# A threshold search without its second product, moved into the first layers of each expert, with w1 in three buffers and the last expert written out

## What is computed

```python
logits = x @ w_gate                      # 3072 x 8
order = np.argsort(-logits.flatten())
for idx in order:                        # greedy: best score first
    tok, e = idx // E, idx % E
    if assigned[tok] >= 0 or counts[e] >= cap: continue
    assigned[tok] = e; counts[e] += 1    # cap = 3072 // 8 = 384
for e in range(E):
    h = np.maximum(x[mask_e] @ w1[e], 0.0)   # w1: 384 x 1024
    out[mask_e] = h @ w2[e]                  # w2: 1024 x 384
y = ((x @ w_a) * (x @ w_b)) @ w_out          # 384 x 1536, 1536 x 384
```

## Time and profile before

| | us |
|---|---|
| median of 3 runs | 1288.75 |
| the profiled execution | 1286.86 |
| its span | 1285.1 |
| PE busy | 1134.4 (88%) |
| DVE busy | 880.1 (68%) |
| POOL busy | 615.1 (48%) |
| ACT busy | 519.2 (40%) |
| attention | about 0 to 420 |
| round 0 alone | about 421 to 483 |
| eight experts | about 483 to 1270 |
| last scatters | 1270.8 to the end |

### The profile page before, as it was taken

The page is one execution under the profiler, slowest core; times in us unless marked ns, Lnnn a source line. Parts: engine busy times, 40 slices in busy tenths (PEclk is TensorE's granted clock), DMA queues, the critical chain, the costliest instruction groups (busy, mean ns, idle before and its releaser), DMA issues.

```text
span 1285.1 us, 38287 instructions
## 1 busy us (share of the span) xinstructions
PE 1134.4 (88%) x14896; PEld 1017.9 (79%) x14896; DVE 880.1 (68%) x1789; ACT 519.2 (40%) x968; POOL 615.1 (48%) x598
## 2 busy tenths in 40 slices
PE   2899999999998319999999999989989999999995
PEld 1577777777777218898988988989889889898894
DVE  6889999999997664765565566565565565575573
ACT  6767777777773213223214214214213213213212
POOL 5667677776664246445145145144235234325322
PEclk8899999999998558999999999999999999999998
DMA  7434334433332350230030030030030021021022
GB/s 117 76 77 85 80 80 87 89 85 82 80 80 64 109 173 26 62 117 0 18 116 0 18 110 6 18 98 18 18 98 18 18 87 29 18 73 43 18 76 59
DMA packets 171359, 81.25 MB, mean 63 GB/s; under 512 B 149680, under 2 KB 161968, under 8 KB 171328
## 3 DMA queue, kind: packets, MB, share of 16 engines
q1 hardware_dynamic: 159568, 42.49, 15.3%
q0 software_dynamic: 11760, 38.35, 9.4%
HBM read 71.38 MB, written 9.44 MB: 63 GB/s over the span
## 4 chain that ended last, share of the span: by engine, by line
PE 53%; DVE 5%; issue 4%; POOL 2%; DMA 1%; ACT 1%; another core or an unknown queue 0%; POOLq 0%; DVEq 0%; ACTq 0%
PE tb L1804 23%; PE acc L1506 7%; PE acc L1507 6%; PE acc L1508 6%; PE tb L1506 3%; PE ps_r L1416 3%; PE tb L1507 2%; PE tb L1508 2%; POOL w_low L1549 2%; DVE slot L1263 1%; DVE ab_low L1730 1%; PE ps_r L1440 1%; DMA xg<-x_rows,tok_g 1%; DVE slot L1379 1%; PE ps_r L1421 1%
## 5 line engine op out<-in xcount | busy, mean ns | idle before, releaser
L1658 ACT CAST ab_high<-ab 128x384 fp32r<-128x384 f32 x96 | 49.3, 514 | 275.0 <-DVE ab L1725 256.4
L1454 POOL COPY row_g<-row_next 128x11 uint32<-128x11 uint32 x9 | 1.7, 189 | 241.1 <-DVE row_next L1354 241.1
L1549 POOL TENSOR_TENSOR w_low<-w1s,w_high 128x384 fp32r<-128x384 f32 x62 | 85.0, 1372 | 58.8 <-ACT w_high L1608 58.8
L1554 POOL TENSOR_TENSOR w_low<-w2s,w_high 128x384 fp32r<-128x384 f32 x64 | 72.7, 1137 | 82.7 <-ACT w_high L1617 82.7
L1506 PE MATMUL acc<-wo_high,ab_high 128*128 128x384 f32 x288 | 102.8, 357 | 5.7 <-DVE ab_low L1730 5.3
L1804 PE MATMUL tb<-x_high,wb_high 128*128 128x384 f32 x288 | 103.4, 359 | 2.1 <-issue 2.0
L1804 PE MATMUL tb<-x_high,wb_low 128*128 128x384 f32 x288 | 99.2, 344 | 3.0 <-issue 3.0
L1507 PE MATMUL acc<-wo_low,ab_high 128*128 128x384 f32 x288 | 99.4, 345 | 0.4 <-issue 0.4
L1508 PE MATMUL acc<-wo_high,ab_low 128*128 128x384 f32 x288 | 98.8, 343 | 0.3 <-issue 0.3
L1654 ACT COPY a_sb<-tb 128x384 f32<-128x384 f32 x96 | 46.0, 479 | 128.1 <-PE tb L1804 68.0
L1804 PE MATMUL tb<-x_high,wa_high 128*128 128x384 f32 x288 | 97.5, 339 | 0.0
(11 more groups left out here) (286 smaller groups left out, 3362.4 us busy)
## 6 DMA issues: line engine op xcount, KB each, us to landing
a_re_in<-in_a_re SPq DMA_DIRECT2D x32, 192.0 KB, 3.3
a_im_in<-in_a_im SPq DMA_DIRECT2D x32, 192.0 KB, 4.1
qk<-in_q SPq DMA_DIRECT2D x26, 192.0 KB, 2.9
qk<-in_k SPq DMA_DIRECT2D x26, 192.0 KB, 3.3
vv<-in_v SPq DMA_DIRECT2D x48, 96.0 KB, 2.8
x_rows<-ysb SPq DMA_DIRECT2D x24, 192.0 KB
w_raw<-in_moe_w_a SPq DMA_DIRECT2D x10, 384.0 KB, 3.4
w_raw<-in_moe_w_b SPq DMA_DIRECT2D x10, 384.0 KB, 3.4
```

The lines of the kernel that those rows point to most:

```text
L1549: nc.gpsimd.tensor_tensor(w1p[1][:, f % 2, :, :], w1_tile(f), w1p[0][:, f % 2, :, :].bitcast(F32), ALU.subtract).then_inc(s["w1_low"], 1)
L1554: nc.gpsimd.tensor_tensor(w2p[1][:, f % 2, :], w2s[:, f, :], w2p[0][:, f % 2, :].bitcast(F32), ALU.subtract).then_inc(s["w2_low"], 1)
```

## The change

- **Search.** `choice` is written four times over (32 columns for each group instead of 8), so the 24 matmuls give 32 rows: the 8 experts four times. DVE marks the thresholds that reach the capacity with their number, takes the maximum (32 x 1), turns the column into a row with a 32 by 32 transpose, takes the maximum again, and writes the new lower bound into the four quarters of the partitions. The second product and the waits on both sides of it are gone. The step widths are made once (`steps`), and the upper bound is worked out after the comparison has been handed to PE. `own` and `need` are new: how many tokens each expert still lacks, on its rows.
- **Place.** The five searches stand after layers 1, 4, 7, 10 and 13 of the expert; the rest follows in the products 1, 2, 3 and 6 (before: layers 1 to 12 and products 1 to 9). The comparison is in two halves everywhere.
- **w1** has three buffers for its halves, and POOL makes w1's low half two tiles ahead of w2's. **The raw buffer** has two parts (before three), to make room.
- **Last expert.** The loop runs 7 times, and the 8th expert is written out behind it without a round, gathers or turning. Its three scatters are issued one behind the other, and only the last wait is left.
- `one_row` (a constant) and `taken` share the tile `running`; POOL makes `own` (a memset and four selects) and `need`, and no `one_row` and `count_e`.

```diff
-NRAW = 3
+NRAW = 2
+NW1 = 3
-ROUTE_LAYERS = (1, 2, 6, 7, 11, 12)
-ROUTE_LAST = ((1, 0), (1, 1), (3, 0), (3, 1), (5, 0), (6, 0), (7, 0), (9, 0))
-PIECES_WITHIN = (1, 0, 1)
-PIECES_AFTER = (1, 1, 1, 1, 2, 3, 1, 2, 1)
-ASKS = 2 * NSEARCH + 4
+ROUTE_LAYERS = (1, 4, 7, 10, 13)
+ROUTE_LAST = ((1, 0), (2, 0), (3, 1), (6, 1))
+PIECES_AFTER = (2, 2, 1, 1, 1, 1, 0, 1)
+ASKS = NSEARCH + 4
...
+    step(pool, g.memset(t["need"][:], float(CAP)))
+    step(pool, g.memset(t["own"][:], 0.0))
+    for turn in range(0, QUAD, E):
+        step(pool, g.affine_select(out=t["own"][:], in_=t["own"][:], compare_op=ALU.not_equal, fill=1.0, base=-turn,
+                                   pattern=[[-1, E]], channel_multiplier=1))
...
-        step(v.tensor_tensor(choice[:], same[:], by_e(free[:]), ALU.mult))
+        step(v.tensor_tensor(choice[:], same[:].unsqueeze(2).broadcast_to([P, G, QUAD // E, E]),
+                             by_e(free[:]).unsqueeze(2).broadcast_to([P, G, QUAD // E, E]), ALU.mult))
...
             answer()
-            ask(v.tensor_scalar(ok_e[:], ps_r[0:E, 0:NTH], count_e[:, 0:1], float(CAP), ALU.add, ALU.is_ge))
+            step(v.scalar_tensor_tensor(marks[:], ps_r[one, 0:NTH], need[one, 0:1], iota[one, 0:NTH],
+                                        ALU.is_ge, ALU.mult))
+            step(v.tensor_reduce(highest, marks[:], AX.X, ALU.max))
+            step(v.transpose(most_rows[:], highest.broadcast_to([QUAD, QUAD])))
+            step(v.tensor_reduce(everywhere, most_rows[:], AX.X, ALU.max))
+            for q in quads:
+                ins = v.tensor_scalar(lows[q, i + 1:i + 2], everywhere, steps[one, i:i + 1], lows[one, i:i + 1],
+                                      ALU.mult, ALU.add)
+            step(ins)
+            if i + 1 < NSEARCH:
+                step(thresholds(v, i + 1))
+                yield n[1]
+                compare(v, i + 1, ask, alone)
+            v.tensor_scalar(over, everywhere, float(NTH - 1), BIG, ALU.is_ge, ALU.mult)
+            step(v.tensor_scalar(above_it, everywhere, 1.0, None, ALU.add))
+            step(v.tensor_scalar(above_it, above_it, steps[one, i:i + 1], lows[one, i:i + 1], ALU.mult, ALU.add))
+            for q in quads if i + 1 == NSEARCH else (one,):
+                ins = v.tensor_scalar(upper[q, i + 1:i + 2], above_it, over, upper[one, i:i + 1], ALU.add, ALU.min)
+            step(ins)
             yield n[1]
-            answer()
-            step(v.tensor_scalar(ok[:], ps_r[:, 0:NTH], 0.5, BIG, ALU.is_ge, ALU.mult))
-            v.tensor_tensor(t1[:], ok[:], thr[:], ALU.add)
-            step(v.scalar_tensor_tensor(t2[:], ok[:], BIG, thr[:], ALU.subtract, ALU.add))
-            v.tensor_reduce(top[:], t1[:], AX.X, ALU.min)
-            step(v.tensor_reduce(bound[:, 0:1], t2[:], AX.X, ALU.max))
-            step(v.tensor_tensor(bound[:, 1:2], bound[:, 1:2], top[:], ALU.min))
...
-                mm = nc.tensor.matmul(ps_r[0:E, 0:NTH], choice[:, g, :], above[:, g, :],
+                mm = nc.tensor.matmul(ps_r[0:QUAD, 0:NTH], choice[:, g, :, :].rearrange("p r e -> p (r e)"),
+                                      above[:, g, :],
                                       start=(g == 0), stop=(g == G - 1))
-            asked()
-            nc.tensor.matmul(ps_r[:, 0:NTH], ones[0:E, :], ok_e[:], start=True, stop=True).then_inc(s["answered"], 1)
...
             def split_weights(p, first=0):
+                for f in range(first, 2):
+                    w1_low(p, f)
                 for f in range(FT1):
+                    if f + 2 < FT1:
+                        w1_low(p, f + 2)
+                    w2_low(p, f)
...
-            gather_next(E - 1, E)
-            scatter(E - 1)
+            take_tokens(E - 1)
+            for i in range(TT):
+                scatter(E - 1, i)
...
-            with pe.Fori(0, E) as p:
-                pieces = route_tensor(pe, pe.snap(p + 1))
+            def expert(p, last):
+                pieces = iter(()) if last else route_tensor(pe, pe.snap(p + 1))
...
+            with pe.Fori(0, E - 1) as p:
+                expert(p, False)
+            expert(E - 1, True)
```

233 lines of the change are left out of this document (124 added, 109 removed).

## The result

The changed kernel takes 1256.92 us (median of 4 runs, 1252.10 to 1259.28), the kernel before 1288.65, measured beside it; the ratio is 0.9756, 95% interval 0.9722 to 0.9791. Forecast was 1237, with a range of 1220 to 1260: the time lies inside that range, 3 us from its end. The profiled execution took 1256.4 us, its span is 1254.4: 30.7 us less than before, where the sum said 52.1.

The account below looks back on a forecast made before the run. PE's chain of waits (53%) was taken as the bound, nearly every PE gap in the experts being time. Eight parts summed to -52.1 us, span 1233.0, forecast 1237 us; own range 1227 to 1246, 8-in-10 range 1220 to 1260.

Parts of the forecast that it names:

- second rival: PE's stalls beside the gathers move with the gathers and stay at their cost: 1255 us; chance 0.22.
- term 6: New waits in the experts as DVE and PE alternate tightly: 0.7 us per expert, +4.9 us (0 to +12).
- Term 1: Search's second product gone in seven experts: -11.2 us; 32 instead of 8 weight columns cost 0 (-1 to +6).
- Term 2: Before hidden 6, PE's 1.36 us wait for POOL's w1 low half goes in seven experts: -9.5 us.
- Term 3: At the expert's end, an earlier comparison removes PE's 0.50 us wait for the last `ab_low`, seven times: -3.5 us.
- Term 4: List product moves behind the gathers, so PE's stalls on issue go in experts 0 to 5: -18.3 us (0 to -28).
- Term 5: Start: POOL's constants +1.6 us, round 0's searches -1.7, later loads through two raw buffers +1.5 (0 to +8).
- third rival: DVE becomes the bound in the first layers, 1 us per search, +35 us: 1272 us; chance 0.12.
- Terms 7 and 8: Last expert without round, turning, gathers or w1 wait: -11.6 us; tail scatters issued back to back: -4.3 us.

Follow-up runs that it names:

- b_last: The kernel before with only the last expert written out behind the loops, its three scatters back to back: 1235.47 us, ratio 0.9865 to the kernel before.
- e_twice: The changed kernel with the four 32 by 1 writes of `lows` done twice in each search: 1307.34 us, ratio 1.0155 to the kernel before.
- e_wide: The changed kernel with `choice` repeated to 128 columns, so one write of `lows` per search replaces four: 1223.63 us, ratio 0.9776 to the kernel before.
- b_both: The kernel before, old search kept, with w1 in three buffers and the last expert written out: 1268.14 us on chip C, ratio 0.9763.

## Why the prediction was right in direction and 20 us too low

The measured 1256.9 us lies outside the forecast's own 1227 to 1246 and beside the second rival's 1255. That nearness is chance: this rival kept PE's stalls at their old price, and in the changed kernel's loop PE has no wait on issue. The time comes from term 6 and the start, less what terms 2, 7 and 8 brought above their forecast.

*Term 1 (second product) held.* L1435 shows no price of 32 columns (0.80 us against 0.79), and the product is gone.

*Term 2 (w1 buffers) was somewhat small*: no wait for `w_low` is left, and alone it gave 13.8 us where I had 9.5 less 1.5 for the loads.

*Term 3 held*: PE's wait for the last `ab_low` is in no row of the loop.

*Term 4 (stalls) was right about PE and missed the others.* The list product lies behind the gathers, and the one wait of PE on issue, 1.3 us at 488.60, is the first layer's behind the turning, which the kernel before has too (1.33 us, for `x_low`). But ACT and DVE still stand still for 3 to 4 us beside the gathers, and in experts 1 and 4 this reaches PE through `slot`, with half clock behind: 97 us instead of 94.2. On chip C the same kernel's stalls reach PE in no expert from 1 on (93.5 to 93.8). I had counted experts 1 to 5 as becoming like 6, and had put the second rival's "DVE has more to do in the products that they now meet" aside. Its size is also a matter of the chip: on B b_last, with the old places, has no such stall, so there was nothing to gain.

*Term 5 (start): +5.1 instead of +1.4.* The order of the asks was seen and under-priced: mended alone it brings 3.2 us. The POOL constants cost less (the four selects 1.20 us for my 2.1), round 0 gave nothing: its searches are 5.28 us apart after 5.33, because answer to comparison is 2.48 us, not 1.8. In expert 0 DVE's work for the ranks collided with the splitting of the second loads: 4.78 us which no term had.

*Term 6 (new waits) is the step that failed.* "I expect no wait to 0.2 us here", and 0.7 an expert in all; it is 4.1. The 1.8 us for the new bound don't follow from their own unit: nine operations at 0.26 are 2.35, and 1.8 is seven, so the four writes "back to back" were counted as two. They cost 1.10 us, the stretch 2.47, and DVE's period became 6.3 where PE's is 5.7. e_twice and e_wide show that this chain is what PE waits for at the searches. It is the third rival at a smaller price: it had 1 us per search; the waits come to 0.5 for each of searches 2 to 4, with `hid_low` behind. The arithmetic stood in the text (5.1, or 5.9 if POOL collides, in 5.7), and most comparisons collide (18 of 30), so the upper number was the one to use. The argument against it, that POOL has only 16 operations of 1 us in 28, was weak: its operations fill 14.1 of the 28 us from 778.6 on. The rule of the Trainium skill cited there ("VectorE: DVE Perf Modes", "Rules for kernel authors": few chained operations) was the right warning; the trace agrees with it, at 0.28 us for each write of 32 x 1.

*Terms 7 and 8 held*: 15.9 forecast, 16.1 alone, and 18.8 in the changed kernel by the turnings.

With the two parts worth 29.9 us on chip B (as a sum) and 31.1 on chip C, the changed kernel's own 31.7 us mean that there the new search came to nearly nothing: what PE's missing stalls gave, DVE's chain took. That split is inferred; b_both was not run beside it.

## What to carry to other kernels

Moving work from the bound engine to another one is paid in the other one's chain: add it up with every small operation at its own measured price, four writes of 32 x 1 being four prices, and with the collided duration where collisions are the rule. A write that must reach all partitions is cheaper made by a wider product (128 columns of weights cost PE nothing here; e_wide's gain is shown on one chip) than by one write per quarter. When the same program takes 1252 and 1299 us on two chips, look where its short instructions meet indirect gathers before comparing anything across chips.

## What the hardware showed

- 24 matmuls of 64 columns took 0.79, 0.80 and 0.71 us with 8, 32 and 128 columns of weights.
- A list product of TensorE that takes 0.62 us took 5.2 beside the gathers on one chip and 0.62 beside them on another, with the same search around it (b_both on C, b_last on B). Why they differ stays open; each chip was measured in one session, so chip and session are not told apart either.
- ACT and DVE waited 3.8, 4.5, 6.2 and 8.2 us beside gathers on something that the profile calls remote; of the 8.2, 6.2 came after the product that DVE needed had ended. That these waits, and PE's on issue, are instructions coming late was only argued.
- An operation on VectorE of 32 x 1 with two scalars from memory took 0.26 us (four in 1.10), of 128 x 1 0.27: 32 or 128 partitions made no difference. A turn of 32 x 32 f32 took 0.20 us. A subtraction of 128 x 24 took 1.80 us beside a GpSimd operation of 768 elements, 0.18 without.
